# Beginning the first ffn one unit of attention earlier, with two places for q, k and the local keys of v

## The reference

```
q_d, k_d, v_d = means of q, k, v over groups of 4 positions
out_d = softmax(q_d k_d^T / 8) v_d, each row repeated 4 times
out_local = softmax(q k^T / 8, only where |i - j| < 4) v
x = out_d + out_local, as 2304 rows of 512
x = prelu(x w_in, alpha) w_out           # 512 -> 2048 -> 512
out = elu(x w2_in) w2_out                # the same sizes
```

## Time and profile before

| | us |
|---|---|
| median of 3 runs | 914.22 (911.05 to 915.74) |
| the profiled execution | 912.4 |
| its span, first to last instruction | 910.6 |
| PE busy in the span | 897.1 (99%) |
| DVE, ACT, POOL busy | 538.1, 299.1, 282.4 |
| first product of the ffn starts | 54.48 |
| first second product starts | 62.70 |

### The profile page before, as it was taken

One profiled execution on the slowest core, in us unless ns is written; L12 is line 12 of the kernel. 1 busy time (PEld: TensorE's weight loads), 2 busy tenths in 40 slices (PEclk: granted clock), 3 DMA queues, 4 the chain that ended last, 5 costly groups with the idle time before them and its releaser, 6 DMA issues.

```text
span 910.6 us, 16928 instructions
## 1 busy us (share of the span) xinstructions
PE 897.1 (99%) x6508; PEld 832.1 (91%) x6508; DVE 538.1 (59%) x1049; ACT 299.1 (33%) x688; POOL 282.4 (31%) x406
## 2 busy tenths in 40 slices
PE   8889999999999999999999999999999999999998
PEld 5779999999999999999999998889888888888887
DVE  6675657555654454464465476566765657665563
ACT  5542324322422132242232233233432325423233
POOL 5689992111201235365376531100011100000000
PEclk9899999999999999999999999999999999999999
DMA  7775532222201125436262254434453444634411
GB/s 155 164 170 148 146 102 68 55 55 55 55 3 27 44 71 166 146 109 189 96 231 70 58 155 113 127 109 119 132 173 116 117 116 116 188 114 118 117 45 70
DMA packets 119840, 100.80 MB, mean 111 GB/s; under 512 B 66001, under 2 KB 82385, under 8 KB 119761
## 3 DMA queue, kind: packets, MB, share of 16 engines
q1 hardware_dynamic: 110512, 93.13, 37.2%
q10 hardware_dynamic: 9248, 6.59, 2.5%
HBM read 80.29 MB, written 19.40 MB: 109 GB/s over the span
## 4 chain that ended last, share of the span: by engine, by line
PE 94%; POOL 2%; issue 1%; DVE 1%; DMA 0%; SPq 0%; ACT 0%; DVEq 0%; POOLq 0%
PE ps L239 29%; PE ps L240 28%; PE ps L241 28%; PE ps L442 1%; PE ps L509 1%; PE ps L466 1%; PE ps L497 1%; PE ps L453 1%; PE ps L474 1%; PE ps L482 1%; POOL p_ls L695 1%; PE ps L1044 0%; DMA qk_nat<-in_k 0%; POOL p_cs L692 0%; PE ps L462 0%
## 5 line engine op out<-in xcount | busy, mean ns | idle before, releaser
L241 PE MATMUL ps<-common,w_hi 128*128 128x384 f32 x768 | 258.2, 336 | 0.0
L240 PE MATMUL ps<-common,w_hi 128*128 128x384 f32 x768 | 258.1, 336 | 0.0
L240 PEld LDWEIGHTS ps<-common,w_hi 128*128 128x128 f32 x768 | 144.6, 188 | 0.0
L241 PEld LDWEIGHTS ps<-common,w_hi 128*128 128x128 f32 x768 | 144.3, 188 | 0.0
L239 PE MATMUL ps<-common,w_out_lo 128*128 128x384 f32 x384 | 132.8, 346 | 0.2 <-DVE common L318 0.2
L239 PE MATMUL ps<-common,w_in_lo 128*128 128x384 f32 x384 | 132.5, 345 | 0.0
L314 ACT ACTIVATE common<-act_g 128x384 fp32r<-128x384 f32 x96 | 50.5, 526 | 242.3 <-PE ps L241 125.6
L872 ACT ACTIVATE act_g<-act_g 128x384 f32<-128x384 f32 x96 | 50.5, 526 | 195.1 <-DVE act_g L868 195.1
L239 PE MATMUL ps<-w_hi,common 128*128 128x512 f32 x288 | 113.6, 394 | 0.0
L241 PE MATMUL ps<-w_hi,common 128*128 128x512 f32 x288 | 113.5, 394 | 0.0
L240 PE MATMUL ps<-w_out_lo,common 128*128 128x512 f32 x288 | 113.5, 394 | 0.0
(11 more groups left out here) (100 smaller groups left out, 1418.7 us busy)
## 6 DMA issues: line engine op xcount, KB each, us to landing
ring<-w_in_parts SPq DMA_DIRECT2D x168, 256.0 KB, 2.7
w_in_parts<-parts SPq DMA_DIRECT2D x8, 1280.0 KB, 5.7
qk_nat<-in_q SPq DMA_DIRECT2D x32, 144.0 KB, 3.1
v_nat<-in_v SPq DMA_DIRECT2D x16, 288.0 KB
out<-xT SPq DMA_DIRECT2D x18, 256.0 KB, 2.2
qk_nat<-in_k SPq DMA_DIRECT2D x30, 144.0 KB, 3.3
v_win<-in_v SPq DMA_DIRECT2D x64, 67.5 KB
raw<-in_moe_w_in SPq DMA_DIRECT2D x16, 256.0 KB, 6.4
```

Source lines behind the costliest of these rows:

```text
L240: pe.matmul(psum, l_hi, r_lo, start=False, stop=False)
L241: return pe.matmul(psum, l_hi, r_hi, start=False, stop=stop)
```

## The change

The job list is written anew. Ahead of the ffn now stand units 0 and 1 (rounds and scores); then for u = 0, 1, 2 the rounds of unit u+2, transposes of u, scores of u+2 and outputs of u; then the transposes of unit 3. Before, it was for u = 0 to 3 transposes of u, scores of u+2, rounds of u+3 and outputs of u. So the scores and rounds of unit 5, the rounds of unit 6 and the outputs of unit 3 move from ahead of the first ffn product to behind it. The leads in the ffn become: outputs of unit 3, transposes of unit 4 and two rounds of unit 5; then its other two rounds. DVE pools these four only behind the low part of chunk 0. Behind that come scores of unit 5, rounds of unit 6, scores of unit 6, rounds of unit 7 and outputs of unit 4, and further on the order is as before. While alone, local scores come ahead of coarse ones, and banks go round over all eight. q, k and the local keys of v of early units get a second place, in parts of `xT` and `act_g` that are not in use yet. The split of weights has a semaphore for w_in and one for w_out, and POOL's list is arranged anew: w_in of chunks 0 and 1 ahead of the probabilities of units 3 and 4, w_out of both behind these.

```diff
+    TRANSPOSES = [("TC", 0), ("TC", 1), ("TL", 0), ("TL", 1)]
+    SCORES, SCORES_BESIDE = [("SL", 0), ("SL", 1), ("SC", 0)], [("SC", 0), ("SL", 0), ("SL", 1)]
     OUTPUTS = [("O", 0), ("O", 1)]
-    STEP = [("TC", 0), ("TC", 1), ("TL", 0), ("TL", 1), *SCORES, *ROUNDS, *OUTPUTS]
-    AHEAD_OF = {"TC": 0, "TL": 0, "O": 0, "SC": 2, "SL": 2, "R": 3}
...
-    order = prologue + [job for u in range(UNITS) for job in step_jobs(u)]
-    ALONE = len(prologue) + BATCH_UNITS * len(STEP)
+    LAST_ALONE = BATCH_UNITS - 1
+    BESIDE = LAST_ALONE + 2
+    def jobs_of(jobs, u):
+        return [(*job, u) for job in jobs] if u < UNITS else []
+    prologue = [job for u in range(2) for job in jobs_of(ROUNDS + SCORES, u)]
+    alone = prologue + [job for u in range(LAST_ALONE) for job in
+                        jobs_of(ROUNDS, u + 2) + jobs_of(TRANSPOSES, u) + jobs_of(SCORES, u + 2) + jobs_of(OUTPUTS, u)]
+    alone += jobs_of(TRANSPOSES, LAST_ALONE)
+    leads = [jobs_of(OUTPUTS, LAST_ALONE) + jobs_of(TRANSPOSES, LAST_ALONE + 1) + jobs_of(ROUNDS[:2], BESIDE),
+             jobs_of(ROUNDS[2:], BESIDE)]
+    beside = [job for u in (BESIDE, BESIDE + 1) for job in jobs_of(SCORES_BESIDE, u) + jobs_of(ROUNDS, u + 1)]
+    beside += jobs_of(OUTPUTS, LAST_ALONE + 1)
+    for u in range(LAST_ALONE + 2, UNITS):
+        beside += jobs_of(TRANSPOSES, u) + jobs_of(SCORES_BESIDE, u + 2) + jobs_of(ROUNDS, u + 3) + jobs_of(OUTPUTS, u)
+    order = alone + sum(leads, []) + beside
...
+    LEAD = [len(jobs) for jobs in leads]
     number = {job: n for n, job in enumerate(order)}
...
-    LEAD = [4, len(SCORES), 1]
...
+    FIRST_BANKS = [*range(4), 4, 5, 6, *range(4), 4, 5, 7, *range(4), 6, 4, 5, 0, 1, 2, 3, 7, 6]
+    RING_OF_BANKS = [4, 5, 0, 1, 2, 3, 7, 6]
+    LEAD_BANKS = [7, 6, *range(4), *range(4)]
     def bank_of(kind, i, u):
         n = number[kind, i, u]
-        if ALONE <= n < ALONE + sum(LEAD):
-            return (3, 0, 1, 2, 3, 7, 6, 7)[n - ALONE]
-        if n >= ALONE:
-            return 6 + (n - ALONE - sum(LEAD)) % 2
-        if u == BATCH_UNITS - 1 and (kind, i) in OUTPUTS:
-            return (7, 6)[i]
-        if kind in ("TC", "TL", "R"):
-            return i + 2 * (kind == "TL")
-        if u < 2 and kind in ("SC", "SL"):
-            return 4 + {("SL", 0): 0, ("SL", 1): 1, ("SC", 0): 2}[kind, i]
-        step, place = (u - 2, SCORES.index((kind, i))) if kind in ("SC", "SL") else (u, OUTPUTS.index((kind, i)) + 1)
-        return 4 + (step + place) % 3
+        if n < len(FIRST_BANKS):
+            return FIRST_BANKS[n]
+        if n < ALONE:
+            return RING_OF_BANKS[(n - len(FIRST_BANKS)) % 8]
+        if n < ALONE + sum(LEAD):
+            return LEAD_BANKS[n - ALONE]
...
+        def behind_outputs_of(u):
+            return number["O", 1, u] + 1
+        first = behind_outputs_of(BATCH_UNITS * (t + 1) - 1) if t else ALONE
+        jobs = order[first:behind_outputs_of(BATCH_UNITS * (t + 2) - 1)]
+        sizes = [] if t else LEAD
         grouped = [jobs[sum(sizes[:n]):sum(sizes[:n + 1])] for n in range(len(sizes))]
...
             if kk == 0:
                 if T == 0:
-                    pe.wait_ge(w_split, c + 1)
...
                 pe.wait_ge(g_split, n + 1)
+                if T == 0:
+                    pe.wait_ge(w_out_split, c + 1)
             if c == 0 and T:
...
+            qk_even = sb("qk_even", [NP, 2, NT, HEADS, D])
+            QK_SETS = LAST_ALONE + 3
+            LOADED_IN = {LAST_ALONE - 1: [], LAST_ALONE: [LAST_ALONE + 3], LAST_ALONE + 1: [LAST_ALONE + 4, LAST_ALONE + 5]}
+            QK_BLOCKS = 2 * NT * HEADS * D // (KC * XW)
...
...
+            def win_place(u):
+                return u % 2 if u < WIN_SETS else 0
...
+            def qk_place(u):
+                return u % 2 if u < QK_SETS else 0
...
-                        exp_local(act, u - 1, 1)
                 elif kind == "TC":
                     copy_pT_coarse(act, u, i)
                 elif kind == "TL":
                     copy_pT_local(act, u, i)
-                elif kind == "SL" and i == 0:
-                    exp_coarse(act, u)
-                elif kind == "SL":
+                elif (kind, i) == ("SL", 1):
                     exp_local(act, u, 0)
-                elif (kind, i) == OUTPUTS[0] and u + 2 == UNITS - 1:
-                    exp_local(act, u + 2, 1)
+                elif kind == "SC" and u < BESIDE:
+                    exp_local(act, u, 1)
+                scored = behind(("SC", 0), n - 1)
+                if scored is not None:
+                    exp_coarse(act, scored)
+                scored = behind(("SL", 1), n - 1)
+                if scored is not None and scored >= BESIDE:
+                    exp_local(act, scored, 1)
+                if (kind, i) == TRANSPOSES[-1] and 1 <= u <= BATCH_UNITS:
+                    act.wait_ge(x_done, 2 * u)
+                    split_x_hi(act, 0, u - 1)
...
+                    if u < BESIDE:
+                        sum_local(dve, u, 0)
                 elif kind == "SL":
                     subtract_max(dve, u, i)
                 elif kind == "R":
-                    pool_round(dve, u, i)
-                    if i == 1:
-                        sum_local(dve, u - 1, 0)
+                    if not ALONE <= n < ALONE + sum(LEAD):
+                        pool_round(dve, u, i)
                 elif kind == "O":
                     if i == 0:
-                        if u + 2 < UNITS:
-                            if u + 3 == UNITS:
-                                sum_local(dve, u + 2, 0)
-                            sum_local(dve, u + 2, 1)
-                            reciprocals(dve, u + 2)
                         copy_coarse(dve, u)
                     write_x(dve, u, i)
+                scored = behind(("SC", 0), n - 3)
+                if scored is not None and scored < BESIDE:
+                    reciprocals(dve, scored)
+                scored = behind(("SL", 1), n - 2)
+                if scored is not None and scored >= BESIDE:
+                    sum_local(dve, scored, 0)
+                scored = behind(("SL", 1), n - 5)
+                if scored is not None and scored >= BESIDE:
+                    sum_local(dve, scored, 1)
+                    reciprocals(dve, scored)
+                for v in range(BATCH_UNITS):
+                    scores = ("SL", 1, v + 3)
+                    if (kind, i, u) == (scores if number[scores] < ALONE else (*TRANSPOSES[-1], v + 1)):
+                        split_x_lo(dve, 0, v)
...
-            EARLY = BATCH_UNITS // 2
...
-                        load_k(sp, u + 4)
-                    if u + 1 < WS:
-                        load_chunk(sp, u + 1)
-                    if u + 1 < UNITS:
+                    if u < 2:
+                        load_chunk(sp, u)
+                    elif u == LAST_ALONE:
+                        load_chunk(sp, 2)
+                    for v in LOADED_IN.get(u, [u + 4]):
+                        had = v - 2 if v <= QK_SETS else v - 1
+                        if v < UNITS:
+                            sp.wait_ge(r_done, 4 * had + 2)
+                            load_q(sp, v)
+                            sp.wait_ge(r_done, 4 * had + 4)
+                            load_k(sp, v)
+                    if u == LAST_ALONE:
+                        load_chunk(sp, 3)
+                    w = u + 2 if u + 2 < WIN_SETS + 1 else u + 1
...
                         sp.wait_ge(o_done, 2 * (u + 1))
-                        load_v_windows(sp, u + 1)
+                        load_v_windows(sp, w)
                 load_q(sp, 0)
-                sp.wait_ge(r_done, 2)
                 load_q(sp, 1)
-                sp.wait_ge(r_done, 4)
                 load_k(sp, 1)
                 load_v_nat(sp, 0)
-                for u in (2, 3):
-                    sp.wait_ge(r_done, 4 * (u - 1) + 2)
-                    load_q(sp, u)
-                    sp.wait_ge(r_done, 4 * (u - 1) + 4)
-                    load_k(sp, u)
-                    if u == 2:
-                        load_v_windows(sp, 0)
-                        load_chunk(sp, 0)
+                sp.wait_ge(r_done, 2)
+                load_q(sp, 2)
+                sp.wait_ge(r_done, 4)
+                load_k(sp, 2)
+                load_v_windows(sp, 0)
+                sp.wait_ge(r_done, 6)
+                load_q(sp, 3)
+                sp.wait_ge(r_done, 8)
+                load_k(sp, 3)
+                load_v_windows(sp, 1)
                 sp.dma_start(alpha_t[:, :], alpha.rearrange("(c p) -> p c", p=P), allow_slow_non_contiguous=True)\
                     .then_inc(alpha_loaded, 16)
...
                             g_lo_part(dve, t, at)
+                            if (t, at) == (0, 0):
+                                for r in range(4):
+                                    pool_round(dve, BESIDE, r)
                         elif what == "split":
...
-                for u in range(BATCH_UNITS):
-                    if u:
```

(44 more changed lines are left out.)

171 lines of the change are left out of this document (90 added, 81 removed).

## The result

The changed kernel took 922.78 us (median of 4 runs, 920.0 to 924.9) beside 913.6 for the kernel before (4 runs): a ratio of 1.010, 95% interval 1.006 to 1.014. Timed again with the experiments it gave 921.31 beside 911.54, ratio 1.0107 (1.0087 to 1.0127). It is slower by 9 to 10 us; the forecast was 914.8, and the time lies above its range. The profiled execution took 922.96 us (span 921.2), 10.6 more than that of before.

What follows compares the result with a forecast made beforehand. TensorE was taken as the bound, nearly gapless from 66 us, so gains lay earlier. 912.4 - 12.0 removed + 10.1 new waits + 2.5 clock = 913.0; +0.6 on the 914.2 median gave 914.8 us, range 907 to 920.5.

Steps and rivals of the forecast that it cites:

- (1): Transfers ahead of the ffn: second places remove unit 3's 2.03 and 0.75 us waits and its outputs' 1.12 us lateness.
- (2): Coarse scores ahead of 66 us: new banks end waits for emptied outputs; with the transfer gains, 8.64 us go.
- (a): Unit 0's transposes and unit 2's local scores: new waits for DVE and ACT, 2.3 us together, bounds 1 and 3.
- (b): Third block of x, in the first ffn products: wait for unit 2's written output, 1.7 us, bounds 0.6 and 2.2.
- (c): Fourth block of x, behind unit 3's outputs in the first lead: wait of 1.1 us, bounds 0.9 and 1.6.
- (d): First second product of the ffn: wait for DVE's low part and pool, 2.2 us, bounds 1.9 and 2.6.
- (e): Coarse scores of unit 5: wait for pools behind ACT's last copies, 0.9 to 1.5 us, taken as 1.2.
- (f): Coarse scores of unit 6, directly behind their last round: wait for copy and pool, charged 1.3 us.
- (g): Stretches of one unit ahead of the ffn: DVE becomes slower than PE, charged 0.3 us for two units.
- the slower rival: Transfers set the pace to unit 3's outputs: v sums late 1.8 us (unit 2), 2.8 (unit 3); 919.4 us, chance 0.22.
- (3): Low clock in 25.50 to 37.30 us goes with the waits before it, -2.9 us; other end, nothing won.
- (h): Clock falls after the new lead waits, onto full ffn products: taken as 2.5 us, bounds 0 and 3.4.

Runs made afterwards that it cites:

- the repeat: The changed kernel without any edit, profiled again and timed with the experiments beside the kernel before: 921.31 us, ratio 1.0107.
- both mends: Changed kernel with the last unit's sums and reciprocals ahead of unit 13's outputs, coarse exponentials from unit 5 right behind their scores: 915.87 us, ratio 1.0040.
- cover and mends: Changed kernel with unit 5's rounds ahead of unit 3's transposes, its scores before the first second product, last-unit sums, reciprocals and coarse exponentials earlier: 914.09 us, ratio 1.0008.
- late begin, mends: Changed kernel with the early ffn begin undone, and last-unit sums, reciprocals and coarse exponentials from unit 6 moved earlier: 909.04 us, ratio 0.9973.

## Why the prediction was wrong

**Removed, (1) and (2), 8.64 us: right.** No wait of the kernel before is left ahead of 66 us.

**Waits charged, 10.1 us: right in sum, with some luck.** Measured in the changed profile against the charge: (a) 0.88 + 0.93 = 1.8 (2.3); (b) 0.2 (1.7), since unit 2's outputs before it were themselves 1.85 us late, and 1.32 in the repeat, where they weren't; (c) 1.08 (1.1); (d) 2.39 (2.2); (e) 0.77 (1.2); (f) 0.29 + 1.15 (1.3). With the 1.85 that is 9.5. So the sum comes out near the charge because a wait that was charged nothing stands in place of (b). (g) shows nowhere; the 0.25 us that the profile gives as idle in three outputs is a keep-busy matmul whose record is missing (the repeat has the record there). What I had as the slower rival's first mechanism, the sum of v for unit 2 late by 1.8 us, came in one of two profiles, but instead of (b) and not on top of it; the rival's other 2.8 us for unit 3 did not come.

**The step that failed first: the list of added waits wasn't complete.** The forecast went through PE's order as far as unit 6's coarse scores and stopped there. The next job in that bank waited for ACT (2.47 us), and at the far end of the list the last unit's reciprocals had moved (2.00 us). Together 4.5 us, both gone once the sums, reciprocals and exponentials were moved; the two mends together gave 6.1. The statement that "the last stretches are full either way" was wrong for the same reason.

**The second: the clock, (3) and (h), -2.9 + 2.5 = -0.4 us.** I took one profile's low stretch as a property of the kernel. The mean granted clock of single runs tells more: 0.9963 over 23 runs of the kernel before, 0.993 over the six of the changed one timed with them. Over those 23 runs the time rose by 0.84 us for each 0.001 of clock less, so 0.0033 is 2.8 us (an estimate), instead of -0.4. The kernel before had 0.9954 and 0.9960 in two other sets of 11 and 29 runs, and by these the term would be 2.0 to 2.5. The low stretch that (3) removes was replaced: in the first profile by one behind the 1.85 us wait, in the repeat by one behind (a), which the forecast had named as the other end of that term. The lead brought the one or two of (h), and the two waits that the list lacked had one more behind each in the first profile (76.2 and 318.5 us), so part of this term belongs to them.

**The sum made anew.** -8.6 of waits, +9.5, +4.5, +2.8 for the clock, -0.5 for the two keep-busy matmuls, +0.3 (at 85.20) and +0.5 for small gaps behind 150 us (5.6 - 3.1 - 2.0): 8.5 of the 9.2 to 9.8 us measured; the rest I can't name. In the repeat the clock fell behind gaps of 0.90 and 0.93 us. The Trainium skill (TensorE: Matmul & The Clock Gate, section "HAM oscillation — how this bites in real kernels") blames long single gaps; the trace does not agree. With the clock up, as by that rule, 5.7 of these 8.5 us would still stand, instead of the 1.9 us won that the forecast had for this case.

**The statement behind the forecast, that the early begin is worth nothing by itself, failed in size.** I had priced its parts (b) to (f), 7.5 us, and set them against gains that do not need it: two places, the banks and the order of the jobs that run alone. The run with the begin undone and the mends has those gains without most of the price (its lead waits 1.60, 0.23 and 0.64 us). The likeliest case in the forecast was a sum of two changes with opposite signs, and the pair should have been judged apart.

Idle time of PE by profile, from 5.41 to 66 us, to 150 us and to the end of the span:

| | to 66 | to 150 | to the end | sum | ratio |
|---|---|---|---|---|---|
| before | 8.6 | 0.0 | 3.1 | 11.7 | 1 |
| changed | 8.7 | 4.4 | 5.6 | 18.7 | 1.0107 |
| both mends | 7.8 | 2.3 | 3.6 | 13.7 | 1.0040 |
| cover and mends | 8.4 | 0.2 | 3.6 | 12.2 | 1.0008 |
| late begin, mends | 4.6 | 0.6 | 3.4 | 8.6 | 0.9973 |

Sums and ratios have one order. Some 0.7 us of the first column in changed, both mends, and cover and mends are the three missing records. The last row is the version that beats both kernels, by 2.5 us the one before.

## What to carry to other kernels

When a job list is written anew, walk it to its end for every engine, and above all at its ends, where jobs are missing: a call placed "five jobs behind" moves when there are no five. For each job ask who had its bank last and what that engine does first; a call one place later can land behind a whole burst. A change that joins a relief (places, banks) with a cost (less cover) is to be priced as two, each against its own undoing. And a stretch of low clock seen in one profile is not a term of a sum: take the mean clock of several runs.

## What the runs showed of the hardware

The places at which the clock fell differed between two profiles of one kernel (38.6, 55.7, 76.2 and 318.5 us in one, 18.9 and 53.1 in the other). A fall followed the two gaps of (a), 0.90 and 0.93 us, in the repeat, and in the first profile the clock stayed at 1.00 behind the same two (0.88 and 0.93). Fifteen keep-busy matmuls in the lead kept the clock there up in a profile, but left the mean of the runs at 0.993. In one run PE stopped for 1.50 us inside a group of 48 matmuls that has no semaphore wait in it, at a DMA share of 0.79.
